# Making the last two block means together on TensorE, spreading all four by GpSimd, and reordering the second unit's turn

## What is computed

```python
k_sum = k.reshape(B, H, nb, block, D).max(axis=3)      # 24 blocks of 32 keys
v_sum = v.reshape(B, H, nb, block, D).mean(axis=3)     # their means: the "means" below
scores_l = scale * np.matmul(q, k.transpose(0, 1, 3, 2))   # only |i - j| < 16 is kept
scores_s = scale * einsum(q, k_sum) + np.log(block)
a = softmax(concatenate([scores_l masked, scores_s]))
out = np.matmul(a, concatenate([v, v_sum]))
...
h = np.maximum(x @ w_in, 0.0);  x = h * h @ w_out                 # 512 -> 2048 -> 512
h = x @ w_in2;  solu = h * softmax(h);  out = layernorm(solu) * g @ w_out2   # 512 -> 1024 -> 512
```

## Time and profile before

| | us |
|---|---|
| median of 3 runs (458.97, 459.83, 460.02) | 459.83 |
| the profiled execution, its whole time | 458.92 |
| its span, first to last instruction | 456.9 |
| TensorE busy | 450.3 (99%) |
| VectorE busy | 260.2 (57%) |
| ScalarE busy | 210.6 (46%) |
| GpSimd busy | 76.1 (17%) |

### The profile page before, as it was taken

One profiled execution on the slowest core, in us unless ns is written; L12 is line 12 of the kernel. 1 busy time (PEld: TensorE's weight loads), 2 busy tenths in 40 slices (PEclk: granted clock), 3 DMA queues, 4 the chain that ended last, 5 costly groups with the idle time before them and its releaser, 6 DMA issues.

```text
span 456.9 us, 6613 instructions
## 1 busy us (share of the span) xinstructions
PE 450.3 (99%) x2470; PEld 370.2 (81%) x2470; DVE 260.2 (57%) x441; ACT 210.6 (46%) x473; POOL 76.1 (17%) x67
## 2 busy tenths in 40 slices
PE   8999999999999999999999999999999999999997
PEld 6778888888888888888888888888888888888885
DVE  3997886976645444344225333345657776767630
ACT  2997666556644444444324333334433345343421
POOL 1411110100000000000000000000134345434510
PEclk9999999999999999999999999999999999999999
DMA  8999598592414621111031111111143333453341
GB/s 289 306 265 268 176 252 236 158 274 60 115 33 138 185 61 44 47 25 23 2 93 53 61 60 57 46 47 47 46 93 74 65 70 69 90 118 71 69 115 46
DMA packets 67903, 49.64 MB, mean 109 GB/s; under 512 B 48160, under 2 KB 52896, under 8 KB 67872
## 3 DMA queue, kind: packets, MB, share of 16 engines
q1 hardware_dynamic: 67872, 49.23, 39.9%
HBM read 33.82 MB, written 5.24 MB: 85 GB/s over the span
## 4 chain that ended last, share of the span: by engine, by line
PE 94%; DVE 2%; DMA 1%; ACT 1%; issue 1%; SPq 0%; POOL 0%; DVEq 0%; ACTq 0%; POOLq 0%
PE bank L1042 29%; PE bank L1070 29%; PE bank L1186 14%; PE bank L1168 14%; PE bank L962 4%; PE bank L1019 3%; DMA q_first<-q_head 1%; PE bank L987 1%; ACT probs L538 1%; DVE probs L745 1%; DVE neg_max L749 1%; PE bank L968 0%; DVE probs L763 0%; POOL k_ext L472 0%; DVE k_sum L720 0%
## 5 line engine op out<-in xcount | busy, mean ns | idle before, releaser
L776 DVE TENSOR_TENSOR sqr<-relu 128x512 f32<-128x512 f32 x48 | 33.1, 689 | 90.5 <-ACT relu L603 90.5
L603 ACT ACTIVATE relu<-bank 128x512 f32<-128x512 f32 x48 | 28.7, 597 | 117.8 <-PE bank L1042 116.8
L1042 PE MATMUL bank<-x_hi,win_hi 128*128 128x512 f32 x192 | 76.5, 398 | 0.0
L1070 PE MATMUL bank<-h_hi,wout_hi 128*128 128x512 f32 x192 | 75.0, 391 | 0.0
L1042 PE MATMUL bank<-x_hi,win_lo 128*128 128x512 f32 x192 | 75.0, 391 | 0.0
L1042 PE MATMUL bank<-x_lo,win_hi 128*128 128x512 f32 x192 | 74.9, 390 | 0.0
L1070 PE MATMUL bank<-h_lo,wout_hi 128*128 128x512 f32 x192 | 74.8, 390 | 0.0
L1070 PE MATMUL bank<-h_hi,wout_lo 128*128 128x512 f32 x192 | 74.8, 389 | 0.0
L522 POOL COPY planes<-cen 128x2048 uint16<-128x2048 uint16 x12 | 33.6, 2799 | 169.5 <-PE bank L1070 113.8
L538 ACT ACTIVATE probs<-probs,neg_max 128x120 f32<-128x120 f32 x96 | 36.6, 382 | 17.4 <-DVE neg_max L749 17.4
L1042 PEld LDWEIGHTS bank<-x_hi,win_lo 128*128 128x128 f32 x192 | 36.1, 188 | 7.5
(11 more groups left out here) (82 smaller groups left out, 708.7 us busy)
## 6 DMA issues: line engine op xcount, KB each, us to landing
win_raw<-w_in_t SPq DMA_DIRECT2D x8, 512.0 KB, 6.3
q_sb<-qT SPq DMA_DIRECT2D x16, 256.0 KB, 4.3
wout_raw<-w_out_t SPq DMA_DIRECT2D x8, 512.0 KB, 6.3
win_raw<-w_t SPq DMA_DIRECT2D x8, 512.0 KB, 3.6
v_ext<-vwin SPq DMA_DIRECT2D x16, 192.0 KB, 4.6
out<-o_sb SPq DMA_DIRECT2D x12, 256.0 KB, 2.9
k_ext<-kT SPq DMA_DIRECT2D x12, 192.0 KB, 4.4
k_raw<-kT SPq DMA_DIRECT2D x4, 400.0 KB, 6.3
```

The source lines that it names most:

```text
L603: nc.scalar.activation(relu[:, :], up_bank(n), ACT.Relu).then_inc(relu_ok, 1)
L776: nc.vector.tensor_tensor(sqr[:, n % 3, :], relu[:, :], relu[:, :], ALU.mult)\
L1042: last = nc.tensor.matmul(up_bank(n), win[a][:, f * WC + k * P:f * WC + (k + 1) * P], x[b][:, c % 2, k * CH:(k + 1) * CH], start=(k == 0 a ...
L1070: last = nc.tensor.matmul(down_bank(d), wout[a][:, f * WC + d * P:f * WC + (d + 1) * P], h[b][:, n % 3, :], start=(f == 0 and a == 0 and b ...
```

## The change

- TensorE: `turned(1)` stands in front of `scores(3)` instead of behind it. `means(2)` (ahead of `scores(4)`) and `means(3)` (behind `turned(3)`) are gone; in their place `means_of_last_two()` stands between `scores(4)` and `scores(5)`. It waits for the copy of the first mean and for both `v_first` transfers, and issues the products of pair 2 and pair 3 in turn, step by step.
- PSUM: pair 2's means stay at partitions 0 to 23 of bank 6, pair 3's move to partitions 64 to 87 of the same bank.
- ScalarE: `copy_mean(p)` copies 24 x 128 elements into `v_ext` (semaphore `vone_ok`), no longer 24 x 1024.
- GpSimd: `spread_mean(p)` copies these into `v_ext_first` eight times over (24 x 1024) and signals `vmean_ok`. Spreads 0 and 1 stand behind `windows_k(5)`, spread 2 behind `windows_k(6)`, spread 3 behind `windows_k(7)`.
- SyncE: `load_vf(3)` is issued ahead of `load_q(8)` and `load_vw_first(0)` instead of behind them.
- `up(0)` and `up(1)`, which reuse the banks, wait for `vone_ok` instead of `vmean_ok`.

```diff
@@ -203,7 +203,7 @@
 
         kwin_ok, ksum_ok, kbc_ok = sem("kwin_ok"), sem("ksum_ok"), sem("kbc_ok")
         vmean_ps, vmean_ok, vsum_ok, vavg_ok = sem("vmean_ps"), sem("vmean_ok"), sem("vsum_ok"), sem("vavg_ok")
-        vkept_ok = sem("vkept_ok")
+        vone_ok, vkept_ok = sem("vone_ok"), sem("vkept_ok")
         scores_ok, masked_ok, max_ok, exp_ok = sem("scores_ok"), sem("masked_ok"), sem("max_ok"), sem("exp_ok")
         den_ok, rec_ok, norm_ok = sem("den_ok"), sem("rec_ok"), sem("norm_ok")
         halves_ok, halves_in = sem("halves_ok"), sem("halves_in")
@@ -253,7 +253,9 @@
             return bank[:, 4 + u % 2 if u < UPC else 6, 0:UQ]
 
         def mean_bank(p):
-            return bank[0:NB, 6 + p % 2, 0:P]
+            if p >= 2:
+                return bank[(p - 2) * QT:(p - 2) * QT + NB, 6, 0:P]
+            return bank[0:NB, 6 + p, 0:P]
 
         def up_bank(n):
             return bank[:, 6 if n == 1 else 7, 0:CH]
@@ -353,9 +355,9 @@
             load_w(win_raw, w_in_t, 0, win_in)
             load_vf(2)
             sp.dma_start(q_first[:, 1, :], q_head[1, :, :]).then_inc(qf_in[2], 16)
+            load_vf(3)
             load_q(UPC)
             load_vw_first(0)
-            load_vf(3)
             load_vw_first(1)
             load_q(UPC + 1)
             load_vw_first(2)
@@ -472,6 +474,13 @@
                 nc.gpsimd.tensor_copy(dst, k_sum[:, p, :].unsqueeze(1).to_broadcast([P, TPU, NB]))\
                   .then_inc(kbc_ok, 1)
 
+            def spread_mean(p):
+                pool.wait_ge(vone_ok, p + 1)
+                src = v_ext[0:NB, p, 0:P].unsqueeze(1).unsqueeze(1).to_broadcast([NB, HPC, TPU, P])
+                cols = slice(p * TPU * P, (p + 1) * TPU * P)
+                nc.gpsimd.tensor_copy(v_ext_first[0:NB, :, cols].rearrange("p h (t d) -> p h t d", t=TPU), src)\
+                  .then_inc(vmean_ok, 1)
+
             def split_probs(u):
                 pool.wait_ge(norm_ok, u + 1)
                 if u > BY_DMA:
@@ -493,8 +502,12 @@
             summaries_k(0, 3)
             windows_k(4)
             windows_k(5)
+            spread_mean(0)
+            spread_mean(1)
             windows_k(6)
+            spread_mean(2)
             windows_k(7)
+            spread_mean(3)
             windows_k(UPC)
             windows_k(UPC + 1)
 
@@ -561,10 +574,7 @@
 
             def copy_mean(p):
                 act.wait_ge(vmean_ps, p + 1)
-                src = mean_bank(p).unsqueeze(1).unsqueeze(1).to_broadcast([NB, HPC, TPU, P])
-                cols = slice(p * TPU * P, (p + 1) * TPU * P)
-                nc.scalar.copy(v_ext_first[0:NB, :, cols].rearrange("p h (t d) -> p h t d", t=TPU), src)\
-                  .then_inc(vmean_ok, 1)
+                nc.scalar.copy(v_ext[0:NB, p, 0:P], mean_bank(p)).then_inc(vone_ok, 1)
 
             def w_in_high(f):
 
@@ -987,12 +997,22 @@
                     last = nc.tensor.transpose(turned_bank(u, t), probs[:, u % 2, t * KX:(t + 1) * KX], ident[:, 0:P])
                 last.then_inc(probsT_ps, 1)
 
+            def means_of_last_two():
+
+                pe.wait_ge(vone_ok, 1)
+                for p in (2, 3):
+                    pe.wait_ge(vf_in[p], 16)
+                for j in range(SK):
+                    at = P + NB - BPK - j * BPK
+                    for p in (2, 3):
+                        last = nc.tensor.matmul(mean_bank(p), ident[:, at:at + NB], v_first[:, p, j * P:(j + 1) * P],
+                                                start=(j == 0), stop=(j == SK - 1), skip_group_check=True)
+                last.then_inc(vmean_ps, 2)
+
             def means(p):
                 if p == 0:
                     pe.wait_ge(ident_in, 16)
                 pe.wait_ge(vf_in[p], 16)
-                if p >= 2:
-                    pe.wait_ge(vmean_ok, p - 1)
                 for j in range(SK):
                     at = P + NB - BPK - j * BPK
                     last = nc.tensor.matmul(mean_bank(p), ident[:, at:at + NB], v_first[:, p, j * P:(j + 1) * P],
@@ -1051,7 +1071,7 @@
                     if n < F1:
                         pe.wait_ge(win_low_ok, n + 1)
                     if n < 2:
-                        pe.wait_ge(vmean_ok, PPB)
+                        pe.wait_ge(vone_ok, PPB)
                     if n >= 2:
                         pe.wait_ge(relu_ok, 1 if n == 2 else n)
                 for k in parts:
@@ -1087,16 +1107,15 @@
             means(1)
             turned(0)
             scores(2)
+            turned(1)
             scores(3)
-            turned(1)
-            means(2)
             scores(4)
+            means_of_last_two()
             scores(5)
             turned(2)
             values(0)
             values(1)
             turned(3)
-            means(3)
             scores(6)
             values(2)
             turned(4)
```

## The result

Over 20 runs each, the changed kernel has a median of 459.78 us (458.87 to 461.03) and the one before 458.84 us (458.14 to 460.33). The ratio is 1.0022 with a 95% interval of 1.0013 to 1.0031: 0.6 to 1.4 us slower, about 1.0. The forecast was a shift of 1.1 us, put on top of 459.83, the median of three runs, which lies 1.0 us above the median of twenty; hence the 460.9 that came out 1.1 too high though the shift is nearly right. The profiled execution (458.92) would have been the better base. That the shift is nearly right says little for its working and is in part luck: the experiments show that the step called the deciding one was not, and a wait that the working leaves out stands beside the one that it has.

A forecast was written before the change was run, and what follows sets the result against it. The prediction took TensorE's feed-forward stretch as the bound, its start set by exps(4); values(0) 1.24 us later moved exps(4) and the end by 1.1, early-turn and copy gains lost, added to 459.83: 460.9 us, range 459.2 to 462.3.

The forecast's parts named there:

- What bounds the kernel: TensorE's long feed-forward stretch: each microsecond it starts later is one at the end; in the head, exps(4)'s start decides.
- Turn 1 ahead of scores 3: TensorE's early turned(1): maxima(3) starts 0.1 us earlier, bounds 0 and 0.66; lost in slack ahead of exps(4).
- Copies: ScalarE's four mean copies: 0.27 us each, shedding 2.9 us in all, worth practically nothing at the end.
- Spreads: GpSimd's four 24 x 1024 spreads: 1.0 us each, nobody waiting; spread 3 hidden by 0.4 us.
- This is the edit that decides: Moving load_vf(3) earlier: it lands at 18.4 us, and load_vw_first(0) at 21.4 instead of 20.2.
- The bytes argument: Transfers land in issue order, so load_vw_first(0) lands when the same bytes are through: 21.4 us instead of 20.2.
- TensorE finishes scores(4) at about 17.5: Before the pair of means: scores(4) follows scores(3) directly, then TensorE waits for load_vf(3) until 18.5 us.
- The sum: Means 18.5 to 20.0, values(0) at 21.6, exps(4) at 23.4; turned(4), turned(5) and the end 1.1 us later.
- The path from values(0) to the end: values(0), 1.24 us later, sets x_high(0) and exps(4) on ScalarE, then turned(4) and turned(5): 1.1 us later.
- no overlap: Rival, 12%: the pair's alternating products take 2.84 us, not 1.5; exps(4) 2.4 us late, time 462.2 us.
- That the move of the transfer is harmless: Rival, 17%: load_vw_first(0) still lands by 20.3 us and load_vf(3) by 17.6; time 459.7 us.
- That what TensorE and ScalarE shed would come off: Rival, 13%: TensorE's and ScalarE's work bounds the head; TensorE's 1.3 us shed come off, time 458.5 us.

The follow-up runs named there:

- weights_late: Changed kernel with windows_k(8) and (9) ahead of spread_mean(3), first w_in transfer behind load_vf(3), both load_q behind load_vw_first(1), w_in casts reordered; ratio to before 1.0048.
- after_again: The changed kernel once more, unaltered, for a second trace; ratio to the kernel before 1.0026.
- means_later: Changed kernel with means_of_last_two() behind scores(5) instead of in front of it; ratio to the kernel before 1.0010.
- turn_only: Kernel before with turned(1) alone moved in front of scores(3); ratio to the kernel before 0.9997.
- spread_only: Kernel before with only ScalarE's short copies and GpSimd's four spreads, TensorE and transfer order as before; ratio to before 1.0008.
- load_only: Kernel before with load_vf(3) alone moved ahead of load_q(8) and load_vw_first(0); ratio to before 1.0003.
- before_hole: Kernel before with one line moved: means(2) behind scores(4) instead of in front of it; ratio to before 1.0004.
- no_wait: Changed kernel without load_vf(3) and the wait for it, so pair 3's means are wrong; ratio to the kernel before 1.0018.
- no_holes: Changed kernel without load_vf(3) and its wait, and q_first of the second four units loaded ahead of load_vf(2); ratio to before 1.0004.

## Why the forecast was near in the shift and wrong in its cause

- **What bounds the kernel**: right in the main. In 14 of the 17 traces the span ends 428.6 to 428.9 us behind the start of turned(5). The other three take longer: weights_late 429.2, with its slow clock, and after_again and means_later 429.4 and 429.6. In these two TensorE waits once more near 82 us, 0.46 and 0.68 us, for a `w_in_low`, which stands in VectorE's list behind a sum over v rows that landed only at 80.4 and 79.9. So an execution can lose half a microsecond to a late transfer outside the head; whether the change makes this more frequent is open (2 of the 10 traces with the pair of means, none of the 7 without it).
- **Turn 1 ahead of scores 3**: right as far as one trace tells, 0.1 us (turn_only; not measurable in the time), and lost in the changed kernel as the forecast said.
- **Copies**: right. 24 x 128 takes 0.25 to 0.26 us, forecast 0.27, and ScalarE's freed time is worth nothing (spread_only).
- **Spreads**: right in price, 1.01 to 1.03 us and 1.43 where one meets normalise(3), wrong in "hidden". I looked at who waits for the spreads and only at windows_k(6) of the copies queued behind them. windows_k(8) and (9), which ran at 19.2 us before, run from 26.6 and from 27.9 in the two traces now, beside normalise(5): 0.2 us on the path.
- **"This is the edit that decides"**: wrong, and the first step that failed. The sum has two prices of the move side by side: load_vf(3) until 18.5 in front of the means, and load_vw_first(0) at 21.4 in front of values(0). The second is in neither chain of the changed kernel (changed, after_again), and load_only, which is the move alone, costs nothing that can be measured (1.0003, 0.6 us at most). The first is real, but only because the means now stand where they have to wait for it. The bytes argument puts the window rows 1.2 us later. Counted from the landing of pair 2's k, they came 7.8 to 8.2 us later in the five traces with the old order and 8.6 to 9.7 in the six with only load_vf(3) moved; the middle values, 8.1 and 8.75, are 0.65 us apart.
- **"TensorE finishes scores(4) at about 17.5"**: wrong, and the second step that failed: it puts the wait for q_first at nothing. scores(4) needs q_first, whose landing at 17.2 stood in the earlier trace rows and was used only as the base for the next transfer. scores(4) starts as q_first lands: at 16.15, 16.99 and 17.38 with landings at 16.1, 17.0 and 17.3 (changed, after_again, before_hole), which is 0.26, 0.27 and 0.63 us of waiting behind the slots before it, up to 0.77 in the other traces. Before, means(2) filled this time: its 1.42 us are ahead of turned(2), and the pair's 1.43 are there too. The pair saves nothing ahead of turned(2); all it saves is means(3)'s slot behind turned(3), where TensorE now waits 1.07 us for x_low(0). The forecast had the second half of this and missed the first.
- **The sum**: the wait for load_vf(3) until 18.5, values(0) at 21.6 and turned(5) at 29.2 came out at 18.54, 21.65 and 29.47 in after_again (whose scores(2) started 0.29 us later than in the trace before; from there on, turned(5) is 1.06 us later). The numbers are near because the last transfer covers both holes: with load_vf(3) at 18.5 it does not matter when scores(4) ran. Without it (no_wait) the middle of the ratio falls by 0.2 to 0.4 us instead of the 1.0 that the working implies.
- **The path from values(0) to the end**: half wrong. It runs by turned(3) and maxima(5), not by x_high(0) and exps(4). exps(4) was at 23.40, as forecast (23.4), but VectorE reaches reciprocals(4) 0.1 us after its end (25.17 against 25.03). The forecast left out that maxima(5) waits for turned(3), which the means set back too.
- **Rivals**: no overlap falls (1.43 us for 24 records). That the move of the transfer is harmless is right by itself as far as load_only can tell, but the loss came elsewhere. That what TensorE and ScalarE shed would come off falls: they shed 1.3 and 2.5 us.

In sum, of about 1.0 us: the holes in front of turned(2) give 0.5 to 1.0 in the two traces, normalise(5) 0.2, and 0.15 come back between turned(2) and turned(4). That the holes are the larger part is shown by the traces, in which the first column grows by just their length, and borne out by the time of no_holes; how it divides between q_first and v_first differs from execution to execution, and before_hole does not settle the share of the first.

## What to carry to other kernels

Work that waits for nothing is worth most where its engine would otherwise stand before a transfer: ask of every group that is moved not what its new place costs, but what the engine does in its old place meanwhile, and read the landing of every operand of the next group. When a copy is put into another engine's list, look at everything queued behind it and what it will then run beside. With landings that move by a microsecond from execution to execution, compare traces from an event that the change doesn't touch, and don't rest a forecast time on three runs: here their median (459.83) was 1.0 us off that of twenty (458.84), and the profiled execution (458.92) was not.

## What was not expected of the hardware

- The same transfers, in the same order, landed up to 1.4 us apart in different executions (mask at 7.1 to 8.5 us), and load_vf(3) of the kernel before at 21.4 and 23.5.
- VectorE's difference of two SBUF tensors took 1.82 us instead of 0.68 beside GpSimd's spread and window copies (weights_late), and GpSimd's spread 1.43 instead of 1.03 beside normalise(3).
- In weights_late TensorE was busy 1.82 of the 4.00 us from 22 to 26, with nothing to do from 24.7 to 26.2. The granted clock was at 0.50 by 26 us and stayed there until 32.
